# Top-32 attention: the threshold from sorted halves of score pairs, and the mask by signs on ScalarE

## What is computed

```python
scores = scale * np.matmul(q, k.transpose(0, 1, 3, 2))
kth = np.partition(scores, -top_k, axis=-1)[..., -top_k:-top_k + 1]
mask = scores >= kth
scores = np.where(mask, scores, -1000000000.0)
scores = scores - np.max(scores, axis=-1, keepdims=True)
attn = np.exp(scores)
attn = attn / (np.sum(attn, axis=-1, keepdims=True) + 1e-09)
return np.matmul(attn, v).astype(np.float32)
```

## Time and profile before

| | |
|---|---|
| Time, median of 3 runs | 1463.44 us (1462.87 to 1472.99) |
| The profiled execution's own time | 1469.82 us |
| Its span in the trace | 1467.9 us |
| Its granted TensorE clock, mean | 0.978 |
| Busy: PE, PEld, DVE, ACT, POOL | 1394.9, 1152.9, 1039.0, 599.4, 571.4 us |

### The profile page before, as it was taken

The page is one execution under the profiler, slowest core; times in us unless marked ns, Lnnn a source line. Parts: engine busy times, 40 slices in busy tenths (PEclk is TensorE's granted clock), DMA queues, the critical chain, the costliest instruction groups (busy, mean ns, idle before and its releaser), DMA issues. The chain is left out here.

```text
span 1467.9 us, 23952 instructions
## 1 busy us (share of the span) xinstructions
PE 1394.9 (95%) x8424; PEld 1152.9 (79%) x8424; DVE 1039.0 (71%) x2142; ACT 599.4 (41%) x1618; POOL 571.4 (39%) x475
## 2 busy tenths in 40 slices
PE   6999999999888999999989999999999999999998
PEld 4777777777676777777779999967777899999997
DVE  7999999999998999999975445556663423422221
ACT  4555555555434665556534434423322212212110
POOL 3666666666755667666512122111221100000001
PEclk9999999999978999999989999999999999999999
DMA  4101110111135434432373853644211112211111
GB/s 119 34 27 34 34 26 19 33 31 30 66 124 193 153 101 138 140 125 81 109 260 127 314 193 125 238 138 137 94 47 59 60 44 72 101 43 44 43 66 43
DMA packets 76558, 141.86 MB, mean 97 GB/s; under 512 B 27083, under 2 KB 27212, under 8 KB 76442
## 3 DMA queue, kind: packets, MB, share of 16 engines
q1 hardware_dynamic: 57994, 88.43, 18.2%
q10 hardware_dynamic: 11120, 29.66, 5.8%
q0 software_dynamic: 7328, 22.28, 4.2%
HBM read 116.75 MB, written 24.65 MB: 96 GB/s over the span
## 5 line engine op out<-in xcount | busy, mean ns | idle before, releaser
L681 POOL TENSOR_SCALAR keep<-s_sb,top 128x576 f32<-128x576 f32 x142 | 244.7, 1723 | 221.2 <-DVE top L708 221.0
L708 DVE MAX8 top<-w_sb 128x8 f32<-128x576 f32 x432 | 305.9, 751 | 0.1
L497 PEld LDWEIGHTS ps_o<-v_sb,eT 128*128 128x128 f32 (+1 forms) x1440 | 188.6, 192 | 57.0 <-issue 45.2
L1944 DVE SCALAR_TENSOR_TENSOR h_lo<-ps_ch,h_hi 128x384 fp32r<-128x384 f32 x96 | 53.4, 556 | 235.8 <-ACT h_hi L1764 235.8
L497 PE MATMUL ps_o<-v_sb,eT 128*128 128x74 f32 (+3 forms) x1440 | 214.4, 287 | 0.0
L710 DVE MATCH_REPLACE8 w_sb<-top,w_sb 128x576 f32<-128x576 f32 x288 | 212.2, 746 | 0.0
L685 POOL TENSOR_TENSOR e_sb<-e_sb,keep 128x576 f32<-128x576 f32 x142 | 200.4, 1412 | 26.4 <-ACT e_sb L603 5.3
L1764 ACT ACTIVATE h_hi<-ps_ch 128x384 fp32r<-128x384 f32 x96 | 47.2, 491 | 280.7 <-PE ps_ch L1548 280.7
L480 PE MATMUL ps_o<-ident 128*128 128x128 f32 x992 | 140.4, 286 | 14.7 <-ACT rows L623 14.7
L480 PEld LDWEIGHTS ps_o<-ident 128*128 128x128 f32 x992 | 125.1, 198 | 21.5 <-ACT rows L623 21.1
L592 ACT ACTIVATE eT<-ps_t 128x512 f32<-128x512 f32 x144 | 86.1, 598 | 129.7 <-PE ps_t L469 125.2
(11 more groups left out here) (322 smaller groups left out, 2348.2 us busy)
## 6 DMA issues: line engine op xcount, KB each, us to landing
w<-in_w SPq DMA_DIRECT2D x18, 2048.0 KB, 14.0
w<-in_w ACTq DMA_DIRECT2D x14, 2048.0 KB, 7.8
stage<-in_w_ch SPq DMA_DIRECT2D x16, 512.0 KB, 4.5
q_sb<-in_q SPq DMA_DIRECT2D x16, 288.0 KB, 3.0
vT<-in_vt SPq DMA_DIRECT2D x16, 288.0 KB, 3.0
x_d<-rows SPq DMA_DIRECT2D x18, 256.0 KB, 3.0
x_d<-u POOLq DMA_DIRECT2D x18, 256.0 KB, 2.6
u<-x_d SPq DMA_DIRECT2D x18, 256.0 KB, 2.8
```

The source lines that it names most:

```text
L497: mm = pe.matmul(ps_o[k % 2][:, lo:hi], eT[k % NT_][0:n, c, :], v_sb[b][0:n, c, lo:hi], start=(c == 0), stop=(c == KC))
L681: pool.tensor_scalar(keep[t % 2][:, :], s_sb[t % NS][:, :], top[t % NS][:, TOPK - 1:TOPK], None, ALU.is_ge).then_inc(s_keep, 1)
L708: dve.max(eight, src).then_inc(s_top, 1)
```

## The change

The two halves of a row of scores are 288 columns each. Of the pairs (column i, column i+288) the larger values form one list (`upper`, on DVE, straight from PSUM), the smaller ones another. The smaller ones are made on POOL with integers: `sums` adds the bit patterns of both halves, `lowers` subtracts the larger. DVE then takes the 32 largest of the upper list (seven operations on 288 columns) and the 16 largest of the lower list (three), and one scan of 17 elements against the reversed second half of the upper list gives the 32nd value. Per pair of tiles DVE now has 20 operations on 288 columns, two `upper`, two scans and three operations on 128 x 2 (`below_kth`), which give a value just below the threshold, negated.

ACT replaces each score in `s_sb` by the sign of its distance to that value (`sign`), POOL multiplies `e_sb` by the sign, and the eviction to `eT` is a Relu, which sets the negative entries to zero. In ACT's body the signs of both tiles of a pair come first, for even t; exp comes ahead of the `eT` eviction. The scores are made one body earlier (LQ 6 for 5). `ps_t4` goes; its transposition uses a part of `ps_o`. `keep_clock` is called once in a body, in front of `turn`. In the middle of the stage SP loads the next head pair's q, k and v ahead of most of the expert weights.

```diff
--- before.py
+++ after.py
...
-    LQ, LE = 5, 2
+    LQ, LE = 6, 2
     MIDDLE = NTILE // 2
     ROUTE, NORM = MIDDLE // 2 + 2, MIDDLE + 3
     HOPS = [(MIDDLE + n, at) for n, at in ((2, 2), (3, 2), (4, 1), (4, 2), (5, 2), (8, 0))]
-    AWAIT = [(ROUTE + n, at) for n, at in ((0, 9), (1, 0), (1, 10), (1, 13), (2, 5), (3, 7))]
-    NS, NE, NT_ = 6, 3, 3
+    AWAIT = [(ROUTE + n, at) for n, at in ((0, 14), (1, 0), (1, 15), (1, 20), (2, 8), (3, 11))]
+    NS, NW, NE, NT_ = 6, 4, 3, 3
+    HALF_TOP = TOPK // 2
+    STEPS = 22
...
-        w_sb = [sb(f"w_sb{n}", [P, S]) for n in range(2)]
-        top = [sb(f"top{n}", [P, TOPK]) for n in range(NS)]
-        nmax = sb("nmax", [P, NE])
+        w_sb = [sb(f"w_sb{n}", [P, S]) for n in range(NW)]
+        top = [sb(f"top{n}", [P, 2, TOPK]) for n in range(2)]
+        nmax = sb("nmax", [P, 2, 2])
+        under = sb("under", [P, 2, 2])
+        ulp = sb("ulp", [P, 2])
+        last = sb("last", [P, 2])
         e_sb = [sb(f"e_sb{n}", [P, S]) for n in range(NE)]
-        keep = [sb(f"keep{n}", [P, S]) for n in range(2)]
...
-        ps_t4 = pb("ps_t4", [P, 512])
+        ps_l = pb("ps_l", [P, 2, 2, HALF_TOP + 1])
...
+            U = 2 * (NPAIR // 4 + 1)
             store_x(0, TPP)
+            sp.wait_ge(s_qk, 2 * TPP * (U - 1) + 1)
+            load_qk(U, 0)
+            load_mid(U, 0)
+            sp.wait_ge(s_vw, U - 1)
+            load_vt(U, 0)
             sp.wait_ge(a["s_idx"], IDX_E)
-            for j in range(2):
-                early_w1(sp, env, j)
-                early_w2(sp, env, j)
-            load_pair(NPAIR // 4 + 1, 0)
+            early_w1(sp, env, 0)
+            sp.wait_ge(s_pv, TPP * (U - 1))
+            load_v(U, 0)
+            early_w2(sp, env, 0)
+            early_w1(sp, env, 1)
+            early_w2(sp, env, 1)
...
+                if k > 0 and h == 0:
+                    pe.wait_ge(s_upper, k)
...
-                pe.transpose(ps_t4[0:S - KC * P, 0:P], e_sb[k % NE][:, KC * P:S], ident[:, :]).then_inc(s_tr, 1)
+                if k == 0:
+                    pe.wait_ge(s_vg, 2)
+                if k >= 2:
+                    pe.wait_ge(s_o, k - 1)
+                pe.transpose(ps_o[k % 2][0:S - KC * P, 384:384 + P], e_sb[k % NE][:, KC * P:S], ident[:, :]).then_inc(s_tr, 1)
...
-                    if 0 < t < EARLY0 and t % 2 == 0:
+                    if 0 < t < EARLY0:
                         keep_clock(t, 4)
                     turn(t)
-                    if t < EARLY0:
-                        keep_clock(t, 4)
...
+            def sign(k):
+                act.wait_ge(s_under, 3 * (k // 2) + 3)
+                act.wait_ge(s_exp, k + 1)
+                act.activation(s_sb[k % NS][:, :], s_sb[k % NS][:, :], ACT.Sign, bias=under[:, (k // 2) % 2, k % 2:k % 2 + 1],
+                               scale=1.0).then_inc(s_sign, 1)
+
+            def exp(k):
+                c, y = k // 2, k % 2
+                if y == 0:
+                    act.wait_ge(s_top, STEPS * c + 2)
+                    act.activation(nmax[:, c % 2, :], top[c % 2][:, :, 0], ACT.Copy, scale=-SCALE).then_inc(s_nm, 1)
+                if k >= NE:
+                    act.wait_ge(s_tr, 2 * (k - NE + 1))
+                act.wait_ge(s_nm, c + 1)
+                act.activation(e_sb[k % NE][:, :], s_sb[k % NS][:, :], ACT.Exp, bias=nmax[:, c % 2, y:y + 1],
+                               scale=SCALE).then_inc(s_exp, 1)
+
+            def evict_scores(k):
+                base, h = k - k % 2, k % 2
+                for n in (base, base + 1):
+                    act.wait_ge(s_qk, 2 * base + 2 * h + n - base + 1)
+                    if h == 0 and n >= NS:
+                        act.wait_ge(s_mask, n - NS + 1)
+                    act.activation(s_sb[n % NS][:, h * SH:(h + 1) * SH], ps_s[n % 2][:, 0:SH], ACT.Copy).then_inc(s_copy, 1)
+
             def body(t):
+                if live(t) and t % 2 == 0 and t < NTILE - 2:
+                    sign(t)
+                    sign(t + 1)
+                if live(t + LE):
+                    exp(t + LE)
...
-                    act.activation(pair[:, 0:KC, :].rearrange("p c q -> p (c q)"), ps_t[:, :], ACT.Copy).then_inc(s_ev, 1)
+                    act.activation(pair[:, 0:KC, :].rearrange("p c q -> p (c q)"), ps_t[:, :], ACT.Relu).then_inc(s_ev, 1)
...
+                if live(t + LQ):
+                    evict_scores(t + LQ)
...
+            def sums(c):
+
+                if not 1 <= c < NTILE // 2:
+                    return
+                pool.wait_ge(s_copy, 4 * c + 4)
+                if c >= 2:
+                    pool.wait_ge(s_top, STEPS * (c - 2) + 12)
+                for k in (2 * c, 2 * c + 1):
+                    w, x = w_sb[k % NW][:, :].bitcast(I32), s_sb[k % NS][:, :].bitcast(I32)
+                    pool.tensor_tensor(w[:, SH:S], x[:, 0:SH], x[:, SH:S], ALU.add).then_inc(s_split, 1)
+
+            def lowers(c):
+
+                if not 1 <= c < NTILE // 2:
+                    return
+                pool.wait_ge(s_upper, 2 * c + 2)
+                pool.wait_ge(s_split, 4 * c - 2)
+                for k in (2 * c, 2 * c + 1):
+                    w = w_sb[k % NW][:, :].bitcast(I32)
+                    pool.tensor_tensor(w[:, SH:S], w[:, SH:S], w[:, 0:SH], ALU.subtract).then_inc(s_split, 1)
...
-                pool.wait_ge(s_top, 14 * (t // 2) + 12 + t % 2 + 1)
-                pool.tensor_scalar(keep[t % 2][:, :], s_sb[t % NS][:, :], top[t % NS][:, TOPK - 1:TOPK], None,
-                                   ALU.is_ge).then_inc(s_keep, 1)
-                pool.wait_ge(s_exp, t + 1)
-                pool.wait_ge(s_keep, t + 2)
-                pool.tensor_tensor(e_sb[t % NE][:, :], e_sb[t % NE][:, :], keep[t % 2][:, :],
-                                   ALU.mult).then_inc(s_mask, 1)
+                if t % 2 == 0:
+                    sums(t // 2 + 2)
+                if live(t) and t < NTILE - 2:
+                    pool.wait_ge(s_exp, t + 1)
+                    pool.wait_ge(s_sign, t + 1)
+                    pool.tensor_tensor(e_sb[t % NE][:, :], e_sb[t % NE][:, :], s_sb[t % NS][:, :], ALU.mult).then_inc(s_mask, 1)
+                if t % 2 == 1:
+                    lowers(t // 2 + 2)
...
+            PLAN = [(step, y, low) for step in range(3) for low in range(2) for y in range(2)]
+            PLAN += [(step, y, 0) for step in range(3, 7) for y in range(2)]
+
+            def upper(k):
+
+                dve.wait_ge(s_copy, 4 * (k // 2) + 3 + k % 2)
+                return dve.tensor_tensor(w_sb[k % NW][:, 0:SH], s_sb[k % NS][:, 0:SH], ps_s[k % 2][:, 0:SH], ALU.max)
+
+            def lower(k):
+
+                return dve.tensor_tensor(w_sb[k % NW][:, SH:S], s_sb[k % NS][:, 0:SH], ps_s[k % 2][:, 0:SH], ALU.min)
...
+                    half = w_sb[(2 * c + y) % NW][:, low * SH:(low + 1) * SH]
+                    first = 8 * (step // 2)
+                    eight = ps_l[:, c % 2, y, 1 + first:9 + first] if low else top[c % 2][:, y, first:first + 8]
+                    if step % 2 == 0:
+                        dve.max(eight, half).then_inc(s_top, 1)
+                    else:
+                        dve.match_replace(out=half, in_to_replace=eight, in_values=half, imm_value=-BIG).then_inc(s_top, 1)
                 else:
-                    dve.wait_ge(s_top, 14 * c + n - 1)
-                rnd, find = n // 4, n % 4 < 2
-                src = s_sb[k % NS][:, :] if n < 4 else w_sb[k % 2][:, :]
-                eight = top[k % NS][:, 8 * rnd:8 * rnd + 8]
-                if find:
-                    dve.max(eight, src).then_inc(s_top, 1)
+                    y = n - 20
+                    dve.wait_ge(s_top, STEPS * c + n - 1)
+                    dve.tensor_tensor_scan(ps_l[:, c % 2, y, :], ps_l[:, c % 2, y, :],
+                                           top[c % 2][:, y, TOPK - 1:HALF_TOP - 2:-1], BIG, ALU.max, ALU.min).then_inc(s_top, 1)
...
+            def below_kth(c, n):
+
+                kth = ps_l[:, c % 2, :, HALF_TOP]
+                if n == 0:
+                    dve.wait_ge(s_top, STEPS * (c + 1))
+                    dve.tensor_scalar(ulp[:, :], kth, -1.0, TINY, ALU.mult, ALU.max).then_inc(s_under, 1)
+                elif n == 1:
+                    dve.wait_ge(s_under, 3 * c + 1)
+                    dve.tensor_tensor(ulp[:, :], ulp[:, :], kth, ALU.max).then_inc(s_under, 1)
                 else:
-                    dve.match_replace(out=w_sb[k % 2][:, :], in_to_replace=eight, in_values=src,
-                                      imm_value=-BIG).then_inc(s_top, 1)
+                    dve.wait_ge(s_under, 3 * c + 2)
+                    dve.scalar_tensor_tensor(under[:, c % 2, :], ulp[:, :], ULP, kth, ALU.mult, ALU.subtract).then_inc(s_under, 1)
...
             for c in range(NTILE // 2):
-                for n in range(14):
+                for n in range(STEPS):
                     top_op(c, n)
                     now[0] = (c, n)
```

(21 more changed lines are left out.)

45 lines of the change are left out of this document (17 added, 28 removed).

## The result

| | before | after |
|---|---|---|
| Time, median of 6 runs each | 1464.64 us (1462.62 to 1472.99) | 1654.11 us (1644.77 to 1660.12) |
| Ratio, 95% interval | | 1.128 (1.1233 to 1.1326) |
| Span of the profiled execution | 1467.9 us | 1651.5 us |
| Mean granted clock | 0.978 | 0.918 |

A forecast was written before the change was run, and what follows sets the result against it. DVE bounds the attention before; after, PE's chain from `values` through sign and multiplication to `turn`. 1463.4 - 18 (first part) + 70 (second part) + 67 (clock) = 1582, given as 1585 us; range 1505 to 1690.

The forecast's parts named there:

- (A): The forecast itself: attention loop paced by PE's wait for the mask, with clock loss, 1585 us; chance 0.50.
- (C): Rival: clock stays down for long in the second part, 1747 us throughout, half 1630; chance 0.14 for over 1650.
- first part: Attention's 41.5 pairs before the early expert units: 9.75 us a pair against 9.66, -18 us; clock +17 us.
- second part: Attention's 29.5 pairs with early expert units: 12.05 us a pair against 9.66, +70 us; clock +50 us.
- upper bounds of DVE and POOL: First part: DVE at 11.0 us a pair would add 52 us, POOL's integer sum at 1.41 us would add 42.
- The chain on ACT: Once a pair, sign waits behind copies of values: 4.00 us from `values` to `turn`, PE idling 2.6 us.
- Both conditions under which the text called itself wrong: Signs start while ACT doesn't wait for `gd`, or PE waits less than 1 us a pair in the second part.
- other signs: Attention profile: clock 0.75 to 0.95 from 460 to 800 us; pairs 9.5 to 10.5 us apart, then 12 to 14.5.
- DVE's sum: DVE's work in the attention: 9.2 us a pair, 0.4 less than before; bounds 8.0 and 11.0.
- POOL's sums: POOL's integer sum of 288 columns in the attention: 885 ns, bounds 0.7 and 1.41 us.
- (B): Rival: attention loop as computed, but the clock holds, 1515 us; chance 0.22.
- The loads: Mid-stage: q and k loaded ahead of most expert weights remove DVE's wait, 5.3 us within the -18.

The follow-up runs named there:

- Experiment 3: Changed kernel with ACT's sign on 288 of 576 columns: 1671.12 us; with six unneeded matmul calls in PE's gap 1566.74 us, with both edits 1576.6 us.
- experiment 1: Changed kernel with ACT's signs ahead of the copies: 1549.76 us; with POOL's sums behind the multiplications: 1648.85 us; with both moves: 1481.39 us.
- both_scores: Changed kernel with signs early, sums late, scores ahead of PE's first slot and later DVE waits in the routing: 1464.33 us, ratio 0.9979.
- fill: Changed kernel with eight unneeded matmuls in front of the turn of even tiles over the whole stage: 1567.54 us, ratio 1.0675.
- experiment 2: The run fill: changed kernel with unneeded matmuls in PE's idle time, order unchanged, 1567.54 us.
- experiment 5: Kernel before with 8 keep_clock matmuls a pair instead of 12: 1467.43 us; kernel before with only SP's new order of loads: 1464.17 us.

## Why the prediction was right, and where its sizes were not

The time, 1654 us for 1585, lies inside the range of 1505 to 1690, and the mechanism is the forecast's: (A), on the way to (C). It also lies above 1650, which the forecast gave a chance of only 0.14, to (C). The stage lost 185.5 us where the sum has 119: 52 of the missing 66 are in the first part, 14 in the second. The range reached so far for other reasons, a share of (C) in the second part or the upper bounds of DVE and POOL, and these bounds did not come; that the first part's error fell inside it is in part luck. By its steps:

**The chain on ACT.** Right. The sign starts 0.11 us behind `rows` (250.29 and 250.40), the multiplication 0.92 after the sign, `turn` 1.46 after that. From the start of `rows` to `turn` the forecast has 0.10 + 0.83 + 1.47 = 2.40 us, the trace 2.49; from even to odd 4.14 and 4.24. Experiment 3 shows the chain in the loop about one to one, experiment 1 that it goes when the order does. Both conditions under which the text called itself wrong stayed away: the signs do wait behind `gd`, and PE waits 3.0 us a pair in the second part (2.5 to 3 forecast). Of its other signs, the clock from 460 to 800 us was 0.80 (0.75 to 0.95 forecast), and the pairs of the second part were 14.2 us apart (12 to 14.5).

**DVE's sum.** Right: the row of MAX8 on the upper list, the replacements and their VALUE_LOAD, and the scan (mean ns behind the busy time):

```profile
L778 DVE MAX8 top<-w_sb 128x8 f32<-128x288 f32 x576 | 232.9, 444 | 0.2
L780 DVE MATCH_REPLACE8 w_sb<-top,w_sb 128x288 f32<-128x288 f32 x432 | 188.9, 442 | 0.0
L780 DVE MATCH_VALUE_LOAD w_sb<-top,w_sb 128x8 f32 x432 | 33.9, 79 | 0.0
L784 DVE TENSOR_TENSOR_SCAN ps_l<-ps_l,top 128x17 f32<-128x17 f32 x144 | 22.8, 190 | 0.0
```

One lasts 0.44 us, but two in a row take 0.81 us, the first of these lines:

```profile
253.57 0.81 DVE L778 MAX8 top<-w_sb 128x8 f32<-128x288 f32 x2
254.29 0.07 DVE L780 MATCH_VALUE_LOAD w_sb<-top,w_sb 128x8 f32 x1
254.35 0.44 DVE L780 MATCH_REPLACE8 w_sb<-top,w_sb 128x288 f32<-128x288 f32 x1
254.71 0.08 DVE L780 MATCH_VALUE_LOAD w_sb<-top,w_sb 128x8 f32 x1
```

The operation behind them starts 0.72 after the first, so a MAX8 costs 0.36 and a replacement with its load 0.42 (254.29 to 254.71). The forecast had 0.36 and 0.43, and 9.2 us a pair against 9.15 measured in `both_scores`. The Trainium skill ("VectorE: DVE Perf Modes", the section on the TRN2 errata) gives a fixed cost of about 150 cycles for each operation. That holds here for the duration of one operation (0.44 us for 288 columns), not for the distance between operations that follow each other; the 11 us a pair that it would have given did not come. The table in that section of the Trainium skill has a second figure, 58 cycles beside the columns; an estimate by it is 346 cycles of 0.96 GHz or 0.36 us for 288 columns, which is the distance that the trace shows. (The prediction counts 25 short operations in its remark on the Trainium skill; by its own list they are 27.)

**POOL's sums.** Forecast 885 ns, with 0.7 and 1.41 us as bounds; they took 793 and 796:

```profile
L702 POOL TENSOR_TENSOR w_sb<-s_sb 128x288 int32<-128x288 int32 x142 | 109.7, 793 | 383.3 <-ACT s_sb L627 379.9 <-DVE ps_l L784 3.4
L712 POOL TENSOR_TENSOR w_sb<-w_sb 128x288 int32<-128x288 int32 x142 | 109.9, 796 | 0.1
```

**First part: the term that failed.** Forecast -18 us and 17 for the clock, so -1; it came to +51.4. A pair at full clock took 10.2 us instead of 9.75, some 19 us over 41.5 pairs. The first `turn` came 4.3 us later than before (25.4 us for 21.1), where the forecast has about 1: 3 us more. The routing was to fit into DVE's slack; it didn't. The signs need DVE's `under` in time, so what DVE does in between can lie on the loop. In `fill`, whose clock in the stretch of the routing (0.86 from 380 to 475 us) was no lower than that of the kernel before (0.84 from 360 to 445 us), that stretch has 14 multiplications in 95 us, and both of these waits:

```profile
PE ps_t L485 <- POOL e_sb L738: 11.1, 7, 5.6
ACT s_sb L609 <- DVE under L800: 10.5, 4, 6.4
```

At 10.2 us a pair the 95 us would hold 9.3 pairs; they hold seven, so some 24 us were lost, where the forecast had 0. The two waits shown are 21.6 us together, on two engines; how much each of them adds is not shown. Last, the clock: `fill` enters the second part at 474.9 us, 18 earlier than after, which is the forecast's 17. These make -18 + 19 + 3 + 24 + 18 = 46 of the 51 us; the other 5 are open. What took the clock's 18 can be seen in after: four pairs before 380 us were 14.0 to 15.3 us long, as from 66.51 us, the `turn` of tile 8, to 81.85, that of tile 10.

**Second part.** Forecast 70 + 50 = 120 us, measured 134. In `fill`, at a clock of 1.00 (0.97 before), the part took 349.8 us (474.9 to the `turn` of tile 142 at 824.7), 64 more than before. So the loop was worth 64 us rather than 70, and the clock 134 - 64 = 70 rather than 50. The loss charged for a stop, 1.7 us, was read from a stop of 1.34 us; with stops of 3 us the loss was 70 / 29.5 = 2.4 a pair.

**The clock as a rule.** The rival (B), a clock that holds, was wrong by the 87 us of experiment 2. The Trainium skill ("TensorE: Matmul & The Clock Gate", Part 1) calls the throttled state the default and advises against long idle gaps. Read as a matter of long gaps alone, it does not agree with this trace: PE's stops for the multiplication in the first part were 1.2 us on average, and 1.5 at most before 380 us, where the clock fell four times; stretches of 40 us there were granted 0.83 to 0.87.

**The loads.** 5.3 us of the sum; alone they moved the time by nothing that can be measured (experiment 5).

## What to carry to other kernels

When a change gives an engine a new operation, look not at how much slack that engine has but at what stands ahead of the operation in its program and what that waits for: here signs of 0.8 us, on an engine that was busy for 60% of the time from 20 to 440 us and 47% from 460 to 800 us, and behind them the sums on POOL, cost most of 190 us, and moving the two gave back 173. PE's stops of 1 to 3 us in each pair cost here nearly as much in clock (87 us) as the longer loop itself (some 100); until the order is mended, unneeded matmuls in the gap are worth their place. And before an engine's work is made shorter, see how full the next one is: with the order mended, DVE's 5% made no measurable difference beside a PE at 96%.
